# Pooled attention and channel mixing on one core: row sums taken one pair later, from double-buffered sums

## The reference

```python
q_pool = q.reshape(B, H, S // factor, factor, D).mean(axis=3)
scores = scale * np.matmul(q_pool, k.transpose(0, 1, 3, 2))
scores = scores - np.max(scores, axis=-1, keepdims=True)
attn = np.exp(scores)
attn = attn / (np.sum(attn, axis=-1, keepdims=True) + 1e-09)
...
xn = (x - mu) / np.sqrt(var + 1e-06) * g_ln
ch = np.maximum(xn @ w_ch1, 0.0) @ w_ch2
return (x + ch).astype(np.float32)
```

## Time and profile before

| | us |
|---|---|
| median of 3 runs | 862.93 (861.38 to 865.47) |
| the profiled execution | 862.46 |
| its span, first to last instruction | 860.6 |
| TensorE busy | 817.8 (95%) |
| VectorE busy | 462.2 (54%) |
| GpSimd busy | 350.8 (41%) |
| ScalarE busy | 329.1 (38%) |
| mean granted clock of TensorE | 0.996 |

### The profile page before, as it was taken

How to read it: one execution, slowest core, us unless ns; L and a number is a source line. 1 busy time by engine, 2 the same in 40 slices (tenths; PEclk the granted TensorE clock), 3 DMA queues, 4 the chain that set the end, 5 groups by cost and what they waited for, 6 DMA issues and landing times.

```text
span 860.6 us, 15910 instructions
## 1 busy us (share of the span) xinstructions
PE 817.8 (95%) x6564; PEld 688.1 (80%) x6564; DVE 462.2 (54%) x711; ACT 329.1 (38%) x709; POOL 350.8 (41%) x248
## 2 busy tenths in 40 slices
PE   6799999999999999999989999999999999999998
PEld 3676777666777667777769999999999999999997
DVE  5788977779887788787525543213223123222111
ACT  1555657555666546575543441121121111121110
POOL 1477888888878778777780000000000000000000
PEclk9999999999999999999999999999999999999999
DMA  5855345553355543430203321001001001001001
GB/s 122 179 148 133 80 102 137 138 121 76 90 126 137 136 100 65 111 83 29 66 14 98 123 73 37 1 1 37 1 1 37 1 1 37 1 1 37 1 1 37
DMA packets 30807, 58.51 MB, mean 68 GB/s; under 512 B 8208, under 2 KB 18704, under 8 KB 27152
## 3 DMA queue, kind: packets, MB, share of 16 engines
q1 hardware_dynamic: 29520, 56.90, 26.5%
q10 hardware_dynamic: 1216, 0.59, 0.3%
HBM read 52.76 MB, written 4.72 MB: 67 GB/s over the span
## 4 chain that ended last, share of the span: by engine, by line
PE 60%; POOL 30%; ACT 4%; issue 2%; DVE 2%; DMA 1%; POOLq 0%; SPq 0%; DVEq 0%; ACTq 0%
POOL acc L424 25%; PE banks L939 23%; PE banks L952 23%; POOL acc L428 5%; PE banks L524 5%; ACT pT L636 3%; PE banks L551 2%; PE banks L471 2%; PE banks L522 2%; DVE pm L726 1%; PE banks L535 1%; PE banks L244 1%; DMA k_in_rows<-in_k_dram 1%; PE banks L443 0%; DVE x L1025 0%
## 5 line engine op out<-in xcount | busy, mean ns | idle before, releaser
L424 POOL TENSOR_TENSOR acc<-acc,pT 128x576 f32<-128x576 f32 x160 | 237.7, 1486 | 23.6 <-ACT pT L636 0.6
L939 PE MATMUL banks<-xT,weights 128*128 128x384 f32 x1152 | 217.1, 338 | 0.0
L952 PE MATMUL banks<-weights,hT 128*128 128x512 f32 x864 | 210.6, 389 | 0.0
L939 PEld LDWEIGHTS banks<-xT,weights 128*128 128x128 f32 x1152 | 202.1, 188 | 6.0 <-issue 0.2
L1008 DVE SCALAR_TENSOR_TENSOR hT<-banks,hT 128x384 fp32r<-128x384 f32 x96 | 53.5, 558 | 271.4 <-ACT hT L989 271.4
L726 DVE TENSOR_REDUCE pm<-banks 128x2 f32<-128x1024 f32 x128 | 153.2, 1223 | 64.6 <-PE banks L471 63.5
L636 ACT ACTIVATE pT<-banks 128x576 f32<-128x576 f32 x288 | 172.1, 653 | 41.2 <-PE banks L522 34.5
L952 PEld LDWEIGHTS banks<-weights,hT 128*128 128x128 f32 x864 | 160.9, 188 | 26.8
L989 ACT ACTIVATE hT<-banks 128x384 fp32r<-128x384 f32 x96 | 47.2, 492 | 323.4 <-PE banks L939 323.4
L524 PE MATMUL banks<-qT,kT 64*128 64x288 f32 x1728 | 163.4, 299 | 4.0 <-DVE kT L711 1.5
L524 PEld LDWEIGHTS banks<-qT,kT 64*128 64x128 f32 x1728 | 135.2, 186 | 19.0 <-DVE pm L726 6.9
(11 more groups left out here) (78 smaller groups left out, 502.6 us busy)
## 6 DMA issues: line engine op xcount, KB each, us to landing
q_in_rows<-in_q_dram SPq DMA_DIRECT2D x56, 284.0 KB, 7.5
k_in_rows<-in_k_dram SPq DMA_DIRECT2D x56, 284.0 KB, 5.2
vn<-in_v_dram SPq DMA_DIRECT2D x16, 576.0 KB, 5.2
wstage<-in_moe_w_ch_dram SPq DMA_DIRECT2D x32, 256.0 KB, 2.8
out_dram<-x SPq DMA_DIRECT2D x16, 256.0 KB, 2.1
k_in_rows<-in_k_dram SPq DMA_DIRECT2D x4, 288.0 KB, 4.8
q_in_rows<-in_q_dram ACTq DMA_DIRECT2D x2, 256.0 KB, 5.0
q_in_rows<-in_q_dram SPq DMA_DIRECT2D x2, 256.0 KB, 3.9
```

The lines of the kernel that those rows point to most:

```text
L424: nc.gpsimd.tensor_tensor(total, pT[:, h % 2, 0] if kt == 1 else total, pT[:, h % 2, kt], ALU.add).then_inc(chained, 1)
L939: last = nc.tensor.matmul(ps_h[f % 2][:, 0:CW], weights[:, 2 * f, a, c * 128:(c + 1) * 128], xT[:, par, b, c], start=m == 0, stop=m == len ...
L952: last = nc.tensor.matmul(ps_y[kk], hT[:, f % 2, a, kk * 128:(kk + 1) * 128], weights[:, 2 * f + 1, b], start=f == 0 and m == 0, stop=f == ...
```

## The change

The row sums `Z` of pair j - 1 are now a step of pair j, between `SH` and the second `PV`, into bank 1. The sums `acc` have two buffers for each half (pair parity), and `add_up` waits for `z_done` one pair further back. Since `z_done` no longer implies that a half of `pT` has been added up, the first exponential of each half waits for `acc_ready` of the half that used its part of `pT` before. Turned sums `E` and outputs `O` are those of pair j - 2. The last pair has a list of its own, `PAIR_END`, with two `E` and two `O`, and VectorE's `VECTOR_END` to match. The row sums of pair 15 are taken in the mix stage behind the first up-projection, its sums and outputs are turned behind the second, and VectorE takes them behind the first activation's low part. `copy_sums`, `take_end` and `scale_outputs` move to the outer level; only what the diff shows changes in them.

```diff
-                  "S@6 M@4 S@0 O@6 E@3 L@0 PV@2 KQ@4 KA@6 T@4 T@5 SH@3 PV@0 Z@2")
+                  "S@6 M@4 S@0 O@6 E@3 L@0 PV@2 KQ@4 KA@6 T@4 T@5 SH@3 Z@1 PV@0")
...
+    PAIR_END = PAIR_STEPS[:PAIR_STEPS.index("O@6")] + "O@6 E@3 Z@5 PV@2 T@4 E@3 O@6 PV@0"
...
+    VECTOR_END = "a e o a t e o"
...
-            elif kind == "Z":
-                yield kind, j, bank
+            elif kind == "Z" and j > 0:
+                yield kind, j - 1, bank
             elif kind == "E":
-                yield kind, j + 1, bank
-            elif kind == "O" and j > 0:
-                yield kind, j - 1, bank
+                yield kind, j + 1 + at, bank
+            elif kind == "O" and j > 1:
+                yield kind, j - 2 + at, bank
...
-    LAST_STEPS = [("E", PAIRS + 1, (6,)), ("O", PAIRS - 1, (2, 3))]
+    LAST_STEPS = [("Z", PAIRS - 1, (2,)), ("E", PAIRS + 2, (6,)), ("O", PAIRS - 1, (2, 3))]
...
-            acc = sb("acc", [128, 2, 2, HW], f32, at)
+            acc = sb("acc", [128, 2, 2, 2, HW], f32, at)
...
-                total = acc[:, h % 2]
-                wait(pool, z_done, h // 2)
+                total = acc[:, h // 2 % 2, h % 2]
+                wait(pool, z_done, h // 2 - 1)
...
-            if n >= 2:
-                pe.wait_ge(z_copied, n - 1)
+            if n >= 3:
+                pe.wait_ge(z_copied, n - 2)
                 last = nc.tensor.transpose(dst[:, 0:128], zs[:], ident[:])
...
-                                            acc[:, at // HW, s, at % HW:at % HW + width],
+                                            acc[:, j % 2, at // HW, s, at % HW:at % HW + width],
...
             def exponential(n):
                 h, kt = n // KT, n % KT
+                if kt == 0:
+                    wait(act, acc_ready, h - 1)
                 act.wait_ge(scored, n + 1)
...
-            take_end(PAIRS + 1)
-            scale_outputs(PAIRS - 1)
...
-                    if isinstance(n, int) and n == 0 and f == 0:
-                        for kind, j, _ in LAST_STEPS:
+                    if isinstance(n, int) and n == 0 and f < 2:
+                        for kind, j, _ in LAST_STEPS[:1] if f == 0 else LAST_STEPS[1:]:
                             tensor_step(pe, kind, j)
...
                     nc.scalar.activation(hT[:, f % 2, 0], ps_h[f % 2][:, 0:CW], ACT.Relu).then_inc(h_hi, 1)
+                    if isinstance(n, int) and n == 0 and f == 0:
+                        copy_sums(PAIRS - 1)
...
                         in1=hT[:, f % 2, 0].bitcast(f32), op0=ALU.max, op1=ALU.subtract).then_inc(h_ready, 1)
+                    if isinstance(n, int) and n == 0 and f == 0:
+                        take_end(PAIRS + 2)
+                        scale_outputs(PAIRS - 1)
```

More of the change, by code:

```diff
@@ L96, in pair_steps @@
         seen = {}
-        for kind, bank in parsed(PAIR_0 if j == 0 else PAIR_STEPS):
+        for kind, bank in parsed(PAIR_0 if j == 0 else PAIR_STEPS if j + 1 < PAIRS else PAIR_END):
             at = seen.get(kind, 0)
@@ L165, in pooled_attention_channel_mix @@
         ATTENTION_WORDS = (2 * KB * DH + QT * 2 * DH + 2 * KT * DH + 2 * 2 * SEQ + 2 * 2 * NQ
-                           + 2 * 128 + 2 * KT * 2 * HW + 3 * 2 * HW + 2 * QW + 2 * 2 * CW)
+                           + 2 * 128 + 2 * KT * 2 * HW + 5 * 2 * HW + 2 * QW + 2 * 2 * CW)
         with ExitStack() as at:
@@ L602, in attention_tensor, with copy_sums, take_end, scale_outputs @@
                     tensor_step(pe, kind, n)
+        def copy_sums(j):
+            nc.scalar.wait_ge(z_done, j + 1)
+            nc.scalar.copy(zs[:], pair_banks("Z", j)[:, 0, 0:128]).then_inc(z_copied, 1)
+        def take_end(n):
+            nc.vector.wait_ge(end_turned, n + 1)
+            dst = pair_banks("E", n)[:, 0]
+            if n < PAIRS:
+                wait(nc.vector, max_ready, n)
+                last = nc.vector.tensor_reduce(pm_rest[:, GROUPS:GROUPS + 1],
+                                               dst[:, 128:128 + SEQ - KEYS_END].unsqueeze(1), AX.X, ALU.max)
+            if n >= 3:
+                wait(nc.vector, sums_inv, n - 3)
+                turned_sums = dst[:, 0:128].rearrange("p (s r) -> p r s", s=2)
+                last = nc.vector.tensor_scalar_add(sums_e[:], turned_sums[:, 0:QT], 1e-9)
+            last.then_inc(end_taken, 1)
+            if n >= 3:
+                nc.vector.wait_ge(end_taken, n + 1)
+                wait(nc.vector, x_written, n - 3)
+                nc.vector.reciprocal(inv[:], sums_e[:]).then_inc(sums_inv, 1)
+        def scale_outputs(j):
+            g = j % BP
+            nc.vector.wait_ge(o_turned, j + 1)
+            nc.vector.wait_ge(sums_inv, j + 1)
+            whole, (_, rows), end_tile = query_slices(j)
+            src = flat(pair_banks("O", j))[:, 0:QW].rearrange("p (t s d) -> p t s d", t=QT, s=2)
+            cols = slice(g * 128, (g + 1) * 128)
+            tile = whole[0][1]
+            nc.vector.tensor_tensor(x[:, tile:tile + FULL, cols].rearrange("p t (s d) -> p t s d", s=2),
+                                    src[:, 0:FULL],
+                                    inv[:, 0:FULL].unsqueeze(3).to_broadcast([128, FULL, 2, DH]), ALU.mult)
+            nc.vector.tensor_tensor(x[rows, end_tile, cols].rearrange("p (s d) -> p s d", s=2),
+                                    src[rows, FULL],
+                                    inv[rows, FULL].unsqueeze(2).to_broadcast([REST, 2, DH]),
+                                    ALU.mult).then_inc(x_written, 1)
         def attention_scalar(act):
@@ L642, in copy_values @@
                 nc.scalar.copy(oT[:, j % 2, c * HW:(c + 1) * HW], pair_banks("PV", h)[:, 0, 0:HW]).then_inc(pv_copied, 1)
-            def copy_sums(j):
-                act.wait_ge(z_done, j + 1)
-                nc.scalar.copy(zs[:], pair_banks("Z", j)[:, 0, 0:128]).then_inc(z_copied, 1)
             def scalar_step(kind, n):
@@ L732, in take_rest @@
                 nc.vector.tensor_reduce(pm_rest[:, 0:GROUPS], pair_banks("L", j), AX.X, ALU.max).then_inc(rest_taken, 1)
[L734 to L751, removed]
             def join_maxima(j):
@@ L763, in join_maxima @@
                 last.then_inc(max_ready, 1)
[L765 to L780, removed]
             def add_end(h):
@@ L821, in attention_vector @@
             for j in range(PAIRS):
-                added = 0
-                for op in VECTOR_STEPS.split():
+                added = ends = outputs = 0
+                for op in (VECTOR_STEPS if j + 1 < PAIRS else VECTOR_END).split():
                     if op == "m" and j + 1 < PAIRS:
@@ L829, in attention_vector @@
                     elif op == "e":
-                        take_end(j + 1)
+                        take_end(j + 1 + ends)
+                        ends += 1
                     elif op == "c" and j + 1 < PAIRS:
                         join_maxima(j + 1)
-                    elif op == "o" and j > 0:
-                        scale_outputs(j - 1)
+                    elif op == "o" and j > 1:
+                        scale_outputs(j - 2 + outputs)
+                        outputs += 1
                     elif op == "Q" and j + TURNED < PAIRS:
```

## The result

The changed kernel takes 838.73 us (median of 4, 836.72 to 840.75) against 863.06 for the kernel before: ratio 0.972, interval 0.968 to 0.976. It is 24.3 us faster. The profiled execution took 840.67 us, span 838.9.

The account below looks back on a forecast made before the run. TensorE and GpSimd wait for each other in turn; the row sums' position makes the period. 19.6 + 2.4 + 1.2 + 0.6 + 1.4 + 2.2 - 0.4 = 27.0 us off 862.46, plus 0.5 to the median: 836.0 us, range 833 to 846.

Parts of the forecast that it names:

- The wait goes whole: Pairs 1 to 14: TensorE's waits before the row sums for GpSimd's last addition vanish, 19.6 us.
- The 24.50 us predicted for a quiet pair: Attention stage: TensorE's own period per pair, 26.20 less 1.53 of wait and 0.17 of restart.
- 19.6 + 2.4 + 0.6 + 1.4 - 0.4: Pairs 1 to 14: wait, restart, pair 1's lost turned sums and outputs, clock dip, less the charge for statistics.
- 0.4 us a pair behind: Pairs 2 to 5: with a weight split GpSimd needs 24.9 us, lags 1.6 in all, and nothing waits for it.
- the statistics: Pair 6: three VectorE statistics of 0.68 us, 2.0 against 1.5 us left, charged once at 0.4 us.
- the first rival: VectorE becomes the partner: its work per pair grows beyond 1.5 us and TensorE waits for its banks; 848 us, chance 0.09.
- the second rival: GpSimd becomes the bound because its additions lengthen beside VectorE's two-input instructions; 872 us, slower, chance 0.03.
- the 1.2 us: Pair 0 loses its row sums, a gain of 1.2 us there, counted back at the end.
- No clock below 1.0 after the first pair: Sign expected in the profile after: TensorE's granted clock never under 1.0 once the first pair is past.
- The dip at 321 us: After a 1.83 us wait TensorE's clock fell to 0.50, losing 1.4 us; taken as gone without the wait.
- The end: From pair 15's first scores, the third up-projection starts at +32.0 instead of +34.2 us: gain 2.2 us.
- sums at half clock (2.29): Last row sums of the kernel before, after a 2.90 us wait, taking 2.29 us at half clock.

Follow-up runs that it names:

- runs 1 and 2: 1: kernel before with doubled sum buffers and new ScalarE wait, row sums unmoved, 863.02 us. 2: changed kernel with one sum buffer per half, 1022.8 us.
- run 3: Both kernels repeated unchanged for second profiles: changed kernel 838.65 us median, kernel before 862.28 us.
- run 4: Changed kernel with GpSimd's four weight splits behind pairs 8 to 11 instead of 2 to 5: 839.84 us.

## Why the prediction was right

It said 836.0 us, 833 to 846; measured 838.73. Its main mechanism was right: the 19.6 us of waits for GpSimd go, because the row sums stand one pair later and have a second buffer (runs 1 and 2). The smaller terms came out less well, and that the total is this near is in part luck. The sum was made against one execution. Its 27.0 us met 21.8 on the profiled executions (862.46 to 840.67), and 22.3 on the second profiles (run 3), whose clocks were alike at the start. By stretches, in us:

| stretch of TensorE | before, first | after, first | gained | before, second | after, second | gained |
|---|---|---|---|---|---|---|
| until pair 1's first matmul | 58.14 | 59.99 | -1.85 | 60.60 | 59.40 | 1.20 |
| pairs 1 to 14 | 367.82 | 346.08 | 21.7 | 366.70 | 345.96 | 20.7 |
| pair 15's first scores to the third up-projection | 34.23 | 32.26 | 2.0 | 32.73 | 32.26 | 0.5 |

- *The wait goes whole.* Right: none is left. The 24.50 us predicted for a quiet pair met 24.51, but by luck: TensorE's own period is 24.36 (run 4), and quiet pairs wait 0.20 us for VectorE, in part hidden, which the prediction had not priced.
- *Pairs 1 to 14.* The sum had 19.6 + 2.4 + 0.6 + 1.4 - 0.4 = 23.6; 21.7 were gained. The 1.9 missing are above all three things. First, four distances with a split, 0.3 each beyond a quiet pair. The prediction had GpSimd "0.4 us a pair behind" and "nothing waits for it". Nothing waits for GpSimd, but VectorE's `acc_end` beside the late additions takes 1.78 us, the next maxima's bank comes free late, and TensorE waits 0.48 us (run 4). Second, the 0.6 us that pair 1 was to gain by losing its turned sums and outputs: without them TensorE reaches the `L` step earlier and waits 0.49 us there for ScalarE's exponential. Third, from pair 12 to 13 it is 24.84 us, 0.3 more than in a quiet pair. Against these, the statistics cost 0.2 us where 0.4 were charged. So the first rival's wait, for a bank that VectorE holds, was real, and its cause was the second rival's, additions that lengthen each other; it was small and at a place where I had not priced it.
- *Pair 0 and the clock.* In the first profiles the 1.2 us are hidden: the low clock lasted to 42 us in the execution after, and pair 1 began 1.85 us later than before. In the second profiles, where both have 0.50 until about 40 us, pair 1 begins 1.20 us earlier, as predicted. "No clock below 1.0 after the first pair" holds, but the start, which I had taken to be the same in both, is where executions differ.
- *The dip at 321 us.* As a term of the sum 1.4 was right, since the 19.6 held a wait there of 1.25 us only. Without the dip the wait is 1.55 (run 3), so the dip itself cost 1.1. It did not come again, and is an accident of one execution.
- *The end.* 2.0 us gained, 2.2 predicted, but 1.5 of them are the second dip, the "sums at half clock (2.29)" of the prediction: against the second profile of the kernel before, the gain is 0.5. The wait for the weight slice was 0.34 us for 0.5. Removing a wait of 2.9 us may well make such a dip rarer; no run tests that.

The medians differ by 24.3 us, 2 more than the second profiles. Single executions lie anywhere from 859.4 to 865.7 before and from 836.6 to 840.8 after, so tenths of the sum can be checked only within a profile.

## What to carry to other kernels

When two engines wait for each other in turn and neither is full, look for the one step whose position closes the circle; move it by one stage and give what it reads a second buffer, both together. Then price what the freed engine now overlaps with: a helper engine that lags by tenths costs through the instructions beside it, even where nobody waits for its result. Before small gains are judged, make the start repeatable; here 23 idle-time transposes did more than a rearranged helper. And take a second profile of the kernel before: dips of the clock in the first one were counted as gains, 1.1 and 1.5 us of 21.8.

## What the runs showed of the hardware

- With gaps in TensorE's first 40 us the granted clock came up for good anywhere from about 30 to 42 us, in unchanged programs; in both second profiles it is recorded as 0.50 from 34 to about 40. In the kernel before, pair 1 began 2.5 us later with it (60.60 for 58.14). With TensorE busy 7.63 of 8 us from 22 to 30 the clock was 1.00 from 30 on in the profiled run, and five runs agreed within 0.7 us.
- In the kernel before, the clock is recorded as 1.00 from the first microsecond, yet its pairs of matmuls with 512 columns take 0.80 us from 14 to 21 us and 0.39 to 0.50 from 33 us on. In the kernel after, such pairs take 0.80 us in the same stretch with a recorded 0.50. So a recorded 1.00 this early need not mean the higher level; the matmuls' durations tell.
- After waits of TensorE of 2.90 and 2.93 us at the same place, the next 24 matmuls took 2.29 us in one execution of the kernel before (granted clock 0.50 at 451 us) and 1.27 in another.
- A three-element VectorE instruction took 0.92 us instead of 0.17 beside a GpSimd one, and an addition of 128x576 anything from 0.75 to 2.02 us.
